# Attention's instruction order on TensorE, ScalarE and VectorE written out group by group, in a fused attention and convolution-gated MLP kernel

## The reference, cut to what matters

```
# attention: q, k, v are (2, 8, 768, 64); block 32, window 16, 24 blocks
k_sum = max of k over each block of 32;  v_sum = mean of v over each block
scores_l = scale * q @ k^T, kept where |i - j| < 16
scores_s = scale * q @ k_sum^T + log(32)
a = softmax(concat(scores_l, scores_s));  x = a @ concat(v, v_sum)
# gated convolution layer, x as (2, 768, 512)
h = relu(x @ w_in); conv_out = 3-tap convolution of h along the tokens
x = (h * sigmoid(conv_out)) @ w_out
# MLP: out = x + relu(layernorm(x) @ w_ch1) @ w_ch2
```

## Time and profile before

| | value |
|---|---|
| three runs, median | 464.88 us (464.83 to 465.04) |
| profiled execution, whole time | 465.05 us |
| its span | 463.3 us |
| PE matmul busy | 453.8 us, 98% |
| DVE busy | 277.6 us, 60% |
| ACT busy | 200.5 us, 43% |
| POOL busy | 270.7 us, 58% |
| granted TensorE clock | 1.00 |

### The profile page before, as it was taken

The page is one execution under the profiler, slowest core; times in us unless marked ns, Lnnn a source line. Parts: engine busy times, 40 slices in busy tenths (PEclk is TensorE's granted clock), DMA queues, the critical chain, the costliest instruction groups (busy, mean ns, idle before and its releaser), DMA issues.

```text
span 463.3 us, 8612 instructions
## 1 busy us (share of the span) xinstructions
PE 453.8 (98%) x3114; PEld 400.3 (86%) x3114; DVE 277.6 (60%) x630; ACT 200.5 (43%) x503; POOL 270.7 (58%) x405
## 2 busy tenths in 40 slices
PE   7899999999999999999999999999999999999997
PEld 6677778988989988989898889998998899889985
DVE  4889886886666978884674643457562334233333
ACT  4989987442334755535333145314220332233210
POOL 2655778999985000087988875890033587878000
PEclk9999999999999999999999999999999999999999
DMA  9999941112202000002115433211020202220003
GB/s 222 205 217 208 230 121 42 52 50 89 68 24 91 1 1 0 1 0 68 50 67 129 121 57 105 91 36 56 38 89 11 93 21 72 91 92 1 1 0 136
DMA packets 74725, 35.28 MB, mean 76 GB/s; under 512 B 57632, under 2 KB 68924, under 8 KB 74684
## 3 DMA queue, kind: packets, MB, share of 16 engines
q1 hardware_dynamic: 71164, 33.85, 27.1%
q10 hardware_dynamic: 3520, 0.88, 0.8%
HBM read 28.83 MB, written 3.15 MB: 69 GB/s over the span
## 4 chain that ended last, share of the span: by engine, by line
PE 89%; DVE 5%; DMA 2%; issue 2%; SPq 1%; ACT 0%; DVEq 0%; ACTq 0%
PE two L1528 10%; PE two L1529 10%; PE two L1527 9%; PE two L1504 9%; PE two L1507 8%; PE two L1506 8%; PE two L1351 5%; PE two L1353 5%; PE two L1352 5%; PE two L1435 5%; PE two L1436 5%; PE two L1434 5%; DVE sm L686 2%; PE two L1336 2%; PE two L1304 1%
## 5 line engine op out<-in xcount | busy, mean ns | idle before, releaser
L604 POOL TENSOR_TENSOR asum<-wst 128x256 f32<-128x256 f32 x26 | 21.8, 839 | 95.4 <-PE two L1353 50.2
L1504 PE MATMUL two<-combo,wa 128*128 128x384 f32 x224 | 75.6, 338 | 0.1
L1507 PE MATMUL two<-combo,wa 128*128 128x384 f32 x224 | 75.4, 337 | 0.0
L1529 PE MATMUL two<-wv,h 128*128 128x512 f32 x192 | 75.3, 392 | 0.0
L1528 PE MATMUL two<-wv,h 128*128 128x512 f32 x192 | 75.2, 392 | 0.0
L1506 PE MATMUL two<-combo,wa 128*128 128x384 f32 x224 | 75.2, 336 | 0.0
L1527 PE MATMUL two<-wv,h 128*128 128x512 f32 x192 | 74.7, 389 | 0.0
L1155 ACT ACTIVATE h<-u 128x384 fp32r<-128x384 f32 x32 | 16.8, 525 | 74.7 <-DVE u L931 67.4
L567 POOL TENSOR_SCALAR pn<-ex,rinv 128x120 f32<-128x120 f32 x96 | 33.5, 369 | 23.9 <-DVE rinv L699 23.9
L598 POOL TENSOR_TENSOR wa<-asum,wa 128x256 fp32r<-128x256 f32 x52 | 43.7, 840 | 4.3
L1504 PEld LDWEIGHTS two<-combo,wa 128*128 128x128 f32 x224 | 42.0, 188 | 2.1 <-issue 0.7
(11 more groups left out here) (119 smaller groups left out, 977.7 us busy)
## 6 DMA issues: line engine op xcount, KB each, us to landing
wst<-in_moe_w_ch SPq DMA_DIRECT2D x26, 512.0 KB, 3.4
vW<-in_v SPq DMA_DIRECT2D x13, 288.0 KB
kn<-in_k SPq DMA_DIRECT2D x15, 192.0 KB, 3.5
qn<-in_q SPq DMA_DIRECT2D x15, 192.0 KB, 3.7
out<-y SPq DMA_DIRECT2D x11, 256.0 KB, 2.0
wst<-in_moe_w_in SPq DMA_DIRECT2D x8, 256.0 KB, 3.3
wst<-in_moe_w_out SPq DMA_DIRECT2D x8, 256.0 KB, 2.9
tok<-xq SPq DMA_DIRECT2D x32, 48.0 KB, 2.0
```

The source lines that it names most:

```text
L1504: nc.tensor.matmul(o, wk[:, 0, kk], ck[:, 0, kk], start=(first and kk == 0), stop=False, skip_group_check=True)
L1507: ins = nc.tensor.matmul(o, wk[:, 1, kk], ck[:, 0, kk], start=False, stop=(kk == 1), skip_group_check=True)
L1529: ins = nc.tensor.matmul(o, lo, vh, start=False, stop=(f == NFP - 1 and c == 1), skip_group_check=True)
```

## The change

The loops over n on PE, ACT and DVE are replaced by lists of single calls, one for each step of each group, and a few calls ahead of the loops change places. No operation is added, removed or resized, POOL's and SP's programs are untouched, and the loads and their order stay as they are. What differs is the order of the calls on three engines: `exps` and `scores` come earlier among the others, `probs_t`, `probs_out` and `outputs` later. The last parts of `hidden(0)` and all of `hidden(1)` now lie ahead of `probs_t(22)`, `taps(0)` ahead of `row_sums(23)`, and `sigmoid(0)` ahead of `relu(1, 0)`. Two waits are added: `window_keys(p)` now waits itself for `keys_t(p)`, since it may now run ahead of `key_max(p)`, and `sigmoid(0)` waits for the last spread means.

The diff, cut to its core:

```diff
@@ window_keys (DVE)
+                dve.wait_ge(ktr_ready, p + 1)
@@ DVE
             score_max(2)
+            row_sums(1)
             means_out(0)
-            row_sums(1)
             key_max(2)
             score_max(3)
+            window_keys(2)
             row_sums(2)
-            window_keys(2)
             score_max(4)
             row_sums(3)
+            score_max(5)
             means_out(1)
-            score_max(5)
+            x_low(0)
             row_sums(4)
...
+            score_max(6)
+            window_keys(3)
+            row_sums(5)
+            score_max(7)
+            key_max(3)
+            row_sums(6)
+            means_out(2)
...
+            row_sums(22)
+            x_low(17)
+            x_low(18)
+            score_max(23)
             dve.wait_ge(cols_done, 1)
             taps(0)
-            x_low(NG - 2)
+            row_sums(23)
+            x_low(19)
+            x_low(20)
             gate(0)
@@ ACT
+            exps(23)
+            probs_out(21)
+            x_high(19)
+            x_high(20)
+            act.wait_ge(v_in[(NPAIR - 1) % 3], v_loads(NPAIR - 1))
+            sigmoid(0)
             relu(1, 0)
+            probs_out(22)
             relu(1, 1)
+            probs_out(23)
@@ PE
+            scores(7)
+            outputs(2)
+            probs_t(4)
             block_means(2)
-            probs_t(4)
+            scores(8)
+            probs_t(5)
+            queries_t(3)
             outputs(3)
...
+            outputs(4)
+            scores(9)
+            block_means(3)
+            keys_t(4)
+            probs_t(6)
+            scores(10)
+            outputs(5)
+            outputs(6)
...
+            probs_t(12)
+            scores(16)
+            probs_t(13)
+            outputs(11)
+            scores(17)
+            queries_t(6)
+            outputs(12)
+            outputs(13)
+            keys_t(7)
+            probs_t(14)
+            scores(18)
+            block_means(6)
...
+            probs_t(20)
+            scores(23)
+            probs_t(21)
+            outputs(19)
+            outputs(20)
             hidden(1, range(KD))
-            outputs(NG - 1)
             hidden(1, range(KD, 2 * KD))
+            probs_t(22)
+            outputs(21)
+            probs_t(23)
+            outputs(22)
+            outputs(23)
```

More of the change, by code:

```diff
@@ L801, in _ @@
-            row_sums(NG - 1)
-            x_low(NG - 4)
-            x_low(NG - 3)
+            score_max(8)
+            x_low(2)
+            x_low(3)
+            row_sums(7)
+            score_max(9)
+            means_out(3)
+            row_sums(8)
+            x_low(4)
+            key_max(4)
+            window_keys(4)
+            score_max(10)
+            row_sums(9)
+            x_low(5)
+            x_low(6)
+            score_max(11)
+            window_keys(5)
+            row_sums(10)
@@ new lines, in _ @@
+            score_max(12)
+            key_max(5)
+            row_sums(11)
+            x_low(7)
+            means_out(4)
+            score_max(13)
+            x_low(8)
+            row_sums(12)
+            score_max(14)
+            x_low(9)
+            row_sums(13)
+            score_max(15)
+            window_keys(6)
+            row_sums(14)
+            score_max(16)
+            key_max(6)
+            means_out(5)
+            row_sums(15)
+            x_low(10)
+            score_max(17)
@@ new lines, in _ @@
+            x_low(11)
+            x_low(12)
+            key_max(7)
+            row_sums(16)
+            score_max(18)
+            means_out(6)
+            window_keys(7)
+            row_sums(17)
+            score_max(19)
+            x_low(13)
+            x_low(14)
+            score_max(20)
+            x_low(15)
+            dve.wait_ge(cols_ready, 1)
+            nc.vector.tensor_copy(cols[:], ps_kq[:, 0:KD + 3 * KF]).then_inc(cols_done, 1)
+            dve.wait_ge(ktr_ready, NPAIR)
@@ L1042, in _ @@
             probs_out(1)
+            queries(2)
             exps(4)
-            queries(2)
             probs_out(2)
             exps(5)
+            x_high(1)
             probs_out(3)
[L1048 to L1068, removed]
+            exps(6)
@@ L1368, in _ @@
             keys_t(2)
+            scores(3)
             probs_t(0)
-            scores(3)
             block_means(1)
@@ L1417, in _ @@
-            probs_t(NG - 1)
+            outputs(4)
[6 more added lines that the diff above has]
+            outputs(6)
+            probs_t(7)
+            queries_t(4)
+            probs_t(8)
+            scores(11)
+            keys_t(5)
+            outputs(7)
+            scores(12)
+            probs_t(9)
+            outputs(8)
+            block_means(4)
+            scores(13)
+            probs_t(10)
@@ new lines, in _ @@
+            queries_t(5)
+            outputs(9)
+            scores(14)
+            probs_t(11)
+            keys_t(6)
+            scores(15)
+            block_means(5)
+            outputs(10)
+            probs_t(12)
[10 more added lines that the diff above has]
+            block_means(6)
+            probs_t(15)
@@ new lines, in _ @@
+            outputs(14)
+            scores(19)
+            outputs(15)
+            probs_t(16)
+            queries_t(7)
+            scores(20)
+            outputs(16)
+            probs_t(17)
+            pe.wait_ge(consts_in, 32)
+            pe.wait_ge(q_done, NPAIR)
+            nc.tensor.transpose(ps_kq[:, 0:KD + 3 * KF], rows[:],
+                                ident[0:KD + 3 * KF, 0:KD + 3 * KF]).then_inc(cols_ready, 1)
+            scores(21)
+            outputs(17)
+            pe.wait_ge(w_done, w_ready("in", 0))
```

118 lines of the change are left out of this document (82 added, 36 removed).

## The result

The changed kernel is slower. Four runs gave 467.36 to 468.59 us, median 468.06; four runs of the kernel before on the same chip gave 464.96. The ratio is 1.0066, 95% interval 1.0049 to 1.0083: 3.1 us more. The profiled execution took 468.31 us with a span of 466.6 at a granted clock of 1.00; TensorE is busy for 452.7 us, VectorE 277.7, ScalarE 200.7, GpSimd 268.6. The work is the same, so the loss is waiting.

The account below looks back on a forecast made before the run. TensorE reaching its gapless part (from 67.5 us) was taken as the bound, then POOL's weight units. TensorE gains 1.8 + 0.1, POOL 2.0; the smaller, 1.9, off the median 464.88 gives 463.0 us, range 461.4 to 465.5.

Parts of the forecast that it names:

- TensorE can win 0.58 us a pair, 1.8 us at 61 us: Attention on TensorE: waits of 0.58 us a pair go, 2.4 us ahead by `outputs(17)`, less 0.6 for loads: 1.8.
- For the other loads I find 1 to 3 us of slack: Loads during attention, other than the keys of pair 7: claimed to have 1 to 3 us in hand.
- the hole at `means_out(1)`: `means_out(1)` moves from 18.74 to 20.2, so SP's loads start 1.1 to 1.6 us later; cost taken as 0.6 us.
- The share of 1.07: DMA engines' share in one pair of heads in mid-attention, read as the transfers filling the DMA engines.
- rival 1: Loads in attention become the pace; late keys of pair 7 shrink the 2.4 us to 0.4: 464.5 us, chance 0.2.
- VectorE's 0.82 us and ScalarE's 0.95: Mid-attention waits in front of `means_out` and, once a pair, `probs_out`, in a ring; the 0.82 us would be filled.
- 37.4 us of work: TensorE's counted work from `probs_t(3)` at 22.31 to 62.45, in 40.1 us, leaving 2.7 us idle.
- The tail on POOL: End of attention: `normalise(23)` 1.3 us earlier plus 1.3 back make unit 19 2.6 us earlier, 2.0 after the loads' 0.6.
- the 1.3 us that I gave back: First weight unit behind attention on POOL: 1.3 us shorter because the taps would no longer lie beside it.
- rival 2: POOL keeps the time: taps hold up split 6 and `normalise(23)`, TensorE waits for unit 19; 464.2 us, chance 0.12.
- Rival 3: Tail jams: `row_sums(23)` waits behind late `taps(0)`, delaying units 8 and 19; slower by 1.4 us, 466.3 us, chance 0.13.
- The two added waits: The waits in front of `window_keys` and `sigmoid(0)`: claimed to cost nothing.

Follow-up runs that it names:

- e4: The changed kernel, but from pair 3 on only 2 of v's 12 blocks are loaded: 463.87 us, ratio 0.9972 to the kernel before.
- e9: Changed order up to `scores(21)`, order of before from there, with 2 of v's 12 blocks loaded from pair 3 on: 463.3 us, ratio 0.9967.
- e13: The changed kernel with a fourth v buffer and all bytes loaded: 467.35 us, ratio 1.0044 to the kernel before.
- e5: The changed kernel with `means_out(1)` back in front of `score_max(5)`: 470.26 us, ratio 1.0117 to the kernel before.
- e7: The kernel before with `means_out(3)` to `means_out(6)` one call later, behind the next `score_max`: 465.53 us, ratio 1.0013.
- e6: The changed kernel with `row_sums(23)` ahead of `taps(0)` on VectorE: 469.45 us, ratio 1.0082 to the kernel before.
- e1: Order of the kernel before up to `outputs(18)` on TensorE, the changed order behind it: 466.25 us, ratio 1.0031 to the kernel before.
- e12: The kernel before with a fourth v buffer, all bytes loaded and orders kept: 465.21 us, ratio 0.9990.
- e11: The changed kernel with `outputs(5)`, `outputs(8)` earlier, `block_means(5)`, `block_means(6)` later on TensorE, and the order of before from `scores(21)` on: 466.12 us, ratio 1.0021.
- e8: The kernel before, each load of v from pair 3 on released one group of outputs later: 468.46 us, ratio 1.0074.
- e2: Changed order up to `scores(21)`, order of the kernel before from there, all loads whole: 470.12 us, ratio 1.0095.

## Why the prediction was wrong

The prediction was 463.0 us, range 461.4 to 465.5; 468.06 came. The sign is wrong, and the time lies outside the range.

- *TensorE can win 0.58 us a pair, 1.8 us at 61 us.* Right as a statement on the order, and shown: e4 and e9 have the forecast's times to 0.2 to 0.7 us, and e9's `project(0)` is 1.8 us earlier.
- *"For the other loads I find 1 to 3 us of slack".* This is the step that failed. Two terms were missing in it. No time from issue to landing of v stands in the prediction, only that of the keys; v takes 7.6 us in the changed kernel. And I held the loads' issue times fixed but for the hole at `means_out(1)`, though the order that I was costing also moves the outputs that release the buffers. The count that was missing: before, the buffer of pair 5 is held from `block_means(5)` at 47.54 to `outputs(17)` at 62.45, 14.9 us; with SyncE's step of some 1 us and 7.6 us of transfer this makes 23.5 us, of the 3 x 8.27 = 24.8 that three buffers have. Slack 1.3 us by this estimate; in the trace v of pair 5 landed 0.7 us ahead of its use. At 3 x 7.69 = 23.1 there is none. What the new order really leaves from release to use is 5.0 to 6.8 us (e4) where before it was 10.2 to 10.4. The slack for v wasn't 1 to 3 us: TensorE waited 3.07 us for v of pair 5, and 1.53 for keys queued behind v.
- *The share of 1.07.* I read it as one point for rival 1 and set against it that SyncE's queue "runs at 7.2 us a pair". That is the pace of issuing. The pace of moving was 8.2 us a pair with the engines full, and nothing in the prediction says how they should follow TensorE to 7.69. e13, where no buffer was missing, still has 2.0 us of waits for loads.
- *Rival 1, the loads become the pace, 464.5, chance 0.2.* The right mechanism at the wrong place: it was priced by one load of keys, pair 7's, and bounded at 2.0 us. It came in pairs 4 and 5 with 4.6 us. It should have been on both sides of the sign.
- *The hole at `means_out(1)`, 0.6 us.* Not confirmed: closing it (e5) gained nothing, because v of pair 3 was then held by `outputs(2)`.
- *VectorE's 0.82 us and ScalarE's 0.95.* I named a ring of waits, but read the gain off their sum. e7 filled the first and the pace stayed at 8.26 and 8.08. (The count behind 37.4 us of work multiplies out to 37.3; nothing hangs on it.)
- *The tail on POOL, 2.6 us earlier.* With the front undisturbed (e4) the hand schedule holds for the taps (70.27, by hand 71.1) and for `normalise(23)` (73.85, by hand 74.1 to 74.3). But e9 with the old tail has 73.86 as well: what the new tail won by its earlier start went into `normalise(22)`, 2.79 us instead of 1.39. And the 1.3 us that I gave back, for taps no longer beside unit 8, didn't come: `gate(0)` took the taps' place and lies beside split 7. In e4 unit 11 ends 1.1 us earlier than before, where TensorE was 3.4 us earlier (82.96), so that it waited 1.92. That is rival 2, POOL keeps the time, by the mechanism which it named, with one more VectorE step in it than I had counted, and at another place: the sum and the rival looked at unit 19 and `project(2)`, but in e4 unit 19 is done at 99.30, 3.8 us earlier than before (103.10), and no wait stands in front of `project(2)`; it is unit 11 and `project(0)` that hold.
- By the rule of the Trainium skill, "SBUF — State Buffer", section "SBUF: two separate sides", VectorE with two SBUF inputs and GpSimd reading SBUF exclude each other for whole instructions. The traces agree: the longest single instruction in `normalise` goes from 0.37 to 1.07 us beside the taps (1.15 and 1.02 us), in the changed kernel and in e6, wherever the taps stand.
- *Rival 3, the tail jams.* With the front of before the kernel is slower by 1.1 us (e1), near the 1.4 that I had priced, but by a link that I hadn't in it: `probs_t(19)` stands behind parts of `hidden(0)`, and POOL waits 1.52 us for it.
- *The two added waits* show in none of the waits of VectorE and ScalarE that I read, as said.

The loss in one sum, by `project(0)`: 86.40, less 1.5 by the better order with its own tail (84.88 in e4), plus 1.53 and 3.07 of waits for transfers, is 89.5; measured 89.96. e4 and e9 are faster only because part of v is left out. A version faster than the kernel before with all its bytes was not found: e12 is equal to it, e11 is 0.2% slower by the median.

## What to carry to other kernels

Before a reordering, make the balance for each ring of buffers: from the call that releases a buffer to the call that wants its new content, in the *new* order, against issue plus transfer; a load that doesn't show in the waits may have 1 us left. The transfer's time is an estimate, since it changes with what else is under way. Where the DMA engines' share is about 1.0, treat the transfers as a bound of their own: here an order that was faster on the compute engines only turned the gain into waits. A wait of 2 us on TensorE may cost nearly twice its length, because the clock can fall behind it.

## What the runs showed of the hardware that I had not expected

- 590 KB of v, in short runs, on nearly full DMA engines took 7.6 us from the second issue to landing in the changed kernel, 7.3 in the kernel before and 5.3 in e8 (each time pair 5), while the keys in the earlier trace rows had a median of 3.3.
- One part of a load can be late by itself: in the changed kernel 31 of 32 parts of v of pair 5 were there at 47.87 and the last at 49.61; in e2 at 48.13 and 49.86.
- Behind idle stretches of TensorE of 1.7 to 3.15 us the granted clock went to 0.59 to 0.67 for some 4 us in some executions and not in others of the same kernel.
